# Chunk-selected attention with a top-capacity expert layer: how the gate row reaches all partitions, and how tokens are ranked against it

## What is computed

```python
q, k, v: (4 batches, 8 heads, 768 positions, 64)
ub = sum(max(q * k_min_of_chunk, q * k_max_of_chunk))   # bound per chunk of 32 keys
top_chunks = argsort(where(causal, ub, -1e9))[..., -6:]
mask = sel & (pos[:, None] >= pos[None, :])
attn = softmax(where(mask, 0.125 * q @ k.T, -1e9))
x = (attn @ v) as (3072 tokens, 512)
probs = softmax(x @ w_gate)                  # 8 experts
expert_idx = argmax; gate_w = probs[token, expert_idx]
for e in range(8):
    tok = the 80 tokens of expert e with the largest gate_w
    out[tok] = gate_w[tok] * (relu(x[tok] @ w1[e]) @ w2[e])   # others stay 0
```

## Time and profile before

| | |
|---|---|
| runs | 292.94 us median (291.65 to 294.74) |
| profiled execution | 292.94 us |
| its span | 291.1 us |
| around the span | 1.8 us |
| PE busy | 275.7 us, 95% |
| POOL busy | 226.5 us, 78% |
| DVE busy | 213.7 us, 73% |
| ACT busy | 147.0 us, 51% |
| TensorE clock granted, mean | 0.988 |

### The profile page before, as it was taken

How to read it: one execution, slowest core, us unless ns; L and a number is a source line. 1 busy time by engine, 2 the same in 40 slices (tenths; PEclk the granted TensorE clock), 3 DMA queues, 4 the chain that set the end, 5 groups by cost and what they waited for, 6 DMA issues and landing times.

```text
span 291.1 us, 8693 instructions
## 1 busy us (share of the span) xinstructions
PE 275.7 (95%) x3606; PEld 169.9 (58%) x3609; DVE 213.7 (73%) x575; ACT 147.0 (51%) x202; POOL 226.5 (78%) x295
## 2 busy tenths in 40 slices
PE   7998999999999999999999999999998999885991
PEld 7554656565656565656564657565655675453661
DVE  5897555566978988759889888898899798811341
ACT  2275655555666454645655555656656554321320
POOL 6079899998999999989999999899969950075232
PEclk9999999999999999999999999999999999998997
DMA  9988999999999999999999979999999799416111
GB/s 149 178 141 142 295 173 204 256 173 168 179 159 167 166 184 170 173 153 187 155 168 155 180 136 188 158 187 171 188 315 148 263 148 196 75 55 128 39 59 60
DMA packets 158359, 47.95 MB, mean 165 GB/s; under 512 B 142405, under 2 KB 150721, under 8 KB 158320
## 3 DMA queue, kind: packets, MB, share of 16 engines
q1 hardware_dynamic: 141664, 28.34, 50.2%
q0 software_dynamic: 13520, 18.67, 40.1%
q10 hardware_dynamic: 3136, 0.39, 0.9%
HBM read 53.49 MB, written 11.01 MB: 222 GB/s over the span
## 4 chain that ended last, share of the span: by engine, by line
PE 65%; POOL 19%; DVE 7%; DMA 3%; issue 3%; ACTq 1%; POOLq 0%; ACT 0%; DVEq 0%
PE SC L509 20%; PE OB L568 18%; POOL ES L554 14%; PE SC L524 4%; PE OB L1136 3%; PE M L595 3%; POOL EXB L545 3%; PE OB L641 3%; PE SC L1112 2%; PE M L472 2%; PE M L581 2%; PE MB L497 2%; DMA qn<-in_q_dram 1%; DMA unsT<-in_moe_w_dram 1%; DMA qn<-x_rows,idx 1%
## 5 line engine op out<-in xcount | busy, mean ns | idle before, releaser
L531 ACT ACTIVATE EXB<-SC 128x1024 f32<-128x1024 f32 x96 | 86.3, 917 | 46.4 <-PE SC L524 45.1
L554 POOL TENSOR_TENSOR ES<-ES,EXB 128x256 f32<-128x256 f32 (+1 forms) x105 | 101.7, 980 | 4.8
L509 PE MATMUL SC<-qT,kT 64*128 64x512 f32 (+3 forms) x512 | 96.3, 466 | 0.1
L568 PE MATMUL OB<-EXB,vn 128*64 128x256 f32 (+3 forms) x704 | 73.0, 361 | 2.1 <-POOL EXB L545 2.1
L568 PEld LDWEIGHTS OB<-EXB,vn 128*64 128x64 f32 x704 | 46.8, 137 | 25.6 <-issue 9.8
L509 PEld LDWEIGHTS SC<-qT,kT 64*128 64x128 f32 x512 | 41.4, 186 | 23.0 <-issue 14.3
L554 POOL TENSOR_TENSOR ES<-EXB 128x768 f32<-128x768 f32 (+1 forms) x30 | 46.6, 1554 | 2.5
L524 PE MATMUL SC<-unsT,ind 64*128 64x128 bf16 (+5 forms) x256 | 37.7, 289 | 0.1
L576 ACT ACTIVATE oT<-OB 128x512 f32<-128x512 f32 (+1 forms) x32 | 15.6, 489 | 40.0 <-PE OB L568 40.0
L545 POOL TENSOR_SCALAR_AFFINE_SELECT EXB<-EXB 128x256 f32<-128x256 f32 x79 | 33.8, 437 | 0.5 <-ACT EXB L531 0.5
L524 PEld LDWEIGHTS SC<-unsT,ind 64*128 64x128 bf16 x256 | 12.8, 95 | 17.8 <-issue 8.0
(11 more groups left out here) (222 smaller groups left out, 418.7 us busy)
## 6 DMA issues: line engine op xcount, KB each, us to landing
w1s<-in_moe_w_dram POOLq DMA_DIRECT2D x8, 1024.0 KB, 10.1
w2s<-in_moe_w_dram POOLq DMA_DIRECT2D x7, 1024.0 KB, 10.8
vn<-in_v_dram SPq DMA_DIRECT2D x32, 192.0 KB, 3.3
kn<-in_k_dram SPq DMA_DIRECT2D x62, 96.0 KB, 3.0
qn<-in_q_dram SPq DMA_DIRECT2D x62, 96.0 KB, 4.0
out_dram<-w1s SPq DMA_DIRECT2D x3, 1536.0 KB, 7.9
x_rows<-xp SPq DMA_DIRECT2D x16, 192.0 KB, 3.5
out_dram<-G SPq DMA_DIRECT2D x1, 1536.0 KB, 10.7
```

What stands on the lines that cost most here:

```text
L509: op("pe", lambda: pe.matmul(o, kT[j][pr, ts(kt)], qT[j][pr, q0:q1], start=True, stop=False), r=[f"kT{j}", f"qT{j}"], w=[f"SC{s}"], inc=False)
L531: op("act", lambda: ac.activation(Ex(st, None, 0, W), src, ACTF.Exp, scale=SCALE), r=[f"SC{s}"], w=[f"E{st}"])
L554: op("gp", lambda: gp.tensor_tensor(o, in0, in1, ALU.add), r=[f"E{s2}", f"E{first[0]}"] if first else [f"E{s2}"] + kt, w=kt)
L568: op("pe", lambda: pe.matmul(OB[pr, q0:q1], vn[s][:, kt, h, :], ex, start=(n == 0), stop=last), r=[f"vn{s}{h}", "ES0" if st is None else f ...
```

## The change

Four things change.

1. The gate row of the first three batches. `gt6` gets 32 columns; `row_out` turns it in blocks of 32 on DVE and SP writes the result to DRAM (128 runs of 128 bytes); `row_in` has SP read the 768 gates back, the same 3 KB for each of 128 partitions. `rank_row`, `rank_pred` and `rank_own` are gone.
2. The comparisons. Tiles are no longer rotated; every batch now uses `diag` (six operations), `low` (columns below the tile, "smaller") and `high` (columns above it, "smaller or equal"), and `count` with 24 matmuls of 192 columns.
3. The index tables. There is one integer tile, `tmp_i`, and five of the seven iotas move into `tables`, each waiting until DVE has read the one before.
4. `last_w2` issues its eight loads at once, in step 15 behind the first two selects.

The core of the diff:

```diff
-                vr, vi = iv(144, 128, [E, NT], [1, E]), iv(192, 128, [1, CAP])
-                op("gp", lambda: gp.iota(vr, pattern=[[0, NT], [-1, E]], base=E, channel_multiplier=0), w=["t0"])
...
                 def tables():
-                    op("dve", lambda: ve.tensor_copy(rank_c[:], vr), r=["t0"], w=["rank_c"])
+                    vr = iv(128, [E, NT], [1, E])
+                    op("gp", lambda: gp.iota(vr, pattern=[[0, NT], [-1, E]], base=E, channel_multiplier=0),
+                       r=["ti"], w=["ti"])
+                    op("dve", lambda: ve.tensor_copy(rank_c[:], vr), r=["ti"], w=["rank_c"])
...
+                def row_out():
+                    op("dve", lambda: ve.transpose(gtT[:], gt6[:]), r=["gt6"], w=["gtT"])
+                    o = bass.AP(gd.tensor, gd.offset, [[32, 4], [128, 32], [1, 32]])
+                    op("sp", lambda: sp.dma_start(o, gtT[:]), r=["gtT"], w=["gd"], dsem="d_gd")
+                def row_in():
+                    a = bass.AP(gd.tensor, gd.offset, [[0, 128], [1, S]])
+                    op("sp", lambda: sp.dma_start(G[:, S:2 * S], a), r=["gd"], w=["grow", "growA", "growB"], dsem="d_gr")
...
+                def diag(b, *jts):
                     for jt in jts:
-                        op("dve", lambda: ve.scalar_tensor_tensor(Cl(jt, jt * 128, 128), triQ[:], gt6[:, jt:jt + 1],
+                        op("dve", lambda: ve.scalar_tensor_tensor(Cl(b, jt, jt * 128, 128), triQ[:], gt6[:, jt:jt + 1],
                                                                   G[:, S + jt * 128:S + (jt + 1) * 128], ALU.mult, ALU.is_ge),
-                           r=["triQ", "gt6"] + gk(jt * 128, jt * 128 + 128), w=[f"D{jt}"])
+                           r=["triQ", "gt6"] + gk(jt * 128, jt * 128 + 128), w=[f"D{jt}"] + Cw(b, jt))
...
                     if i == NP - 1:
-                        last_w2(range(4))
+                        last_w2()
                     if live and kk == 1:
-                        rank_pred()
-                        rank_cmp(bb, 5)
+                        low(bb, 5)
                     if live and kk == 2:
-                        rank_count(bb)
+                        count(bb, (5, 0, 4, 1, 3, 2))
                     if live and kk == 0:
                         gate_exp()
                         gate(bb)
+                        row_out()
                     if i + 2 < NP:
                         take_k(i + 2)
+                    if live and kk == 0:
+                        row_in()
                     if i + 4 < NP:
                         load(i + 4, "qk")
                     if live and kk == 1:
-                        rank_diag(bb)
-                        rank_cmp(bb, 4, 3, 2, 1, 0)
+                        diag(bb, *range(NT))
+                        for jt in (0, 4, 1, 3, 2):
+                            if jt:
+                                low(bb, jt)
+                            high(bb, jt)
                     if i + 1 < NP:
                         unselT(i + 1)
-                    if live and kk == 0:
-                        rank_row(bb)
```

More of the change, by code:

```diff
@@ L268, in _body @@
                 lsum = al(pers, "lsum", [128, NT])
-                gt6 = al(pers, "gt6", [128, NT])
+                gt6 = al(pers, "gt6", [128, 32])
+                gtT = al(pers, "gtT", [128, 32])
                 G = al(pers, "G", [128, 2 * S])
@@ L349, in _body, with iv @@
                 M0b = bass.AP(M0, 0, [[512, 128], [1, 512]]).bitcast(BF16)
-                def iv(off, rows, *dims):
-                    return bass.AP(G, off, [[2 * S, rows]] + [list(d) for d in dims]).bitcast(I32)
+                def iv(rows, *dims):
+                    return bass.AP(tmp_i, 0, [[160, rows]] + [list(d) for d in dims])
                 def load(i, what="qkv", eng="sp", gs=range(4)):
@@ L776, in last_count @@
                                                        start=(n == 0), stop=(n == NT - 1)),
[L777 removed]
+                               r=["ohb", f"D{jt}"] + ([f"L{jt}"] if jt else []) + ([f"U{jt}"] if jt < NT - 1 else []) + Cw(b, jt),
                                w=["MB"], inc=(n == NT - 1 and c == 3))
                         keep_warm(warmth[n])
[L781 to L793 removed]
                 def rank_slot(b):
@@ L917, in fill, with last_w2 @@
                     op("sp", lambda: sp.dma_start(zd, zs), r=[zk], w=[f"outz{g}"], dsem=f"d_zero{g}")
-                def last_w2(fbs):
-                    for fb in fbs:
+                def last_w2():
+                    for fb in range(FB):
                         src = bass.AP(moe_w2.tensor, moe_w2.offset + ((E - 1) * Fd + fb * 128) * Dm, [[Dm, 128], [1, Dm]])
@@ L1045, in _body @@
                 values(NP - 1, (1,), (1, 9), False)
-                last_high(0)
-                last_low(5, "act")
+                high(b, 0)
+                low(b, 5, "act")
                 values_out(1)
-                last_low(4, "act")
-                last_low(3, "act")
-                last_diag(0, 1, 2, 3, 4, 5)
-                last_low(1, "dve")
-                last_high(1)
+                low(b, 4, "act")
+                low(b, 3, "act")
+                diag(b, 0, 1, 2, 3, 4, 5)
+                low(b, 1, "dve")
+                high(b, 1)
                 rows(NP - 1)
                 keep_warm(4)
-                last_high(4)
-                last_high(3)
-                last_low(2, "dve")
-                last_high(2)
+                high(b, 4)
+                high(b, 3)
+                low(b, 2, "dve")
+                high(b, 2)
                 scale_rows(NP - 1)
                 gate_gcols(b)
-                last_count((0, 5, 1, 4, 2, 3), (0, 0, 0, 0, 0, 6))
+                count(b, (0, 5, 1, 4, 2, 3), (0, 0, 0, 0, 0, 6))
                 rank_slot(b)
@@ L1158, in _body @@
                 gather(4)
-                last_w2((4, 5))
                 for e in range(1, E):
```

104 lines of the change are left out of this document (33 added, 71 removed).

## The result

The changed kernel takes 311.06 us (median of 4 runs, 309.89 to 311.52) beside 292.29 us (290.05 to 294.74): 1.066 times the time before, 95% interval 1.059 to 1.074. Its profiled execution took 311.52 us with a span of 309.6 us, 18.5 us more than before.

The account below looks back on a forecast made before the run. PE was taken to set the pace, with POOL nearly as busy. Start +3.5, ranks +11.5 and experts -3.8 us sum to +11.2 us: span 302.3, time 304.1, said as 304; the range ran from 293 to 312 us.

Parts of the forecast that it names:

- start: Before step 0's values: five iotas waiting on DVE's table operations delay POOL's first select, and PE; +3.5 us (2.3 to 4.7).
- ranks, first batch: Steps 4 to 6: late row and fifteen comparisons meeting POOL's adds make PE wait 4.8 us at the count; +6.2 us.
- ranks, second: Second batch: SP less behind, row 1.0 us late in place of 2.9, PE's wait at the count 3.9 us; +4.3 us.
- ranks, third: Third batch: POOL waits 2.1 us for a zero fill, during which no add holds DVE; +1.0 us.
- experts: Second weights of expert 7, issued at once: wait and slow matmuls go, select and gather slightly later; -3.8 us (-5 to -2).
- The even odds on the clock: Behind PE's wait at the start, the clock may fall, 1.5 us more for the matmuls; at even odds 0.7 us.
- Comparisons that take 1 to 2 us beside adds: Expected sign on DVE: rank comparisons that meet POOL's adds wait for them and take 1 to 2 us.
- a wait of PE at the count for DVE of 4 to 5 us: Expected sign in step 6, first batch: PE stands 4 to 5 us at the count until DVE's comparisons end.
- less in step 10, little in step 14: Expected sign: PE's wait at the count, 4 to 5 us in step 6, shrinks in the second and third batch.
- DVE hides the fifteen ops: Rival, count in a batch's second step: comparisons end before PE needs them, each batch saves 0.8 us; 290 us, chance 0.14.
- The early loads hold what they should free: Rival, step 15: the eight weight loads hold POOL or the gathers, spending the 3.8 us gain; 308 us, chance 0.20.
- Every row is late: Rival, all three batches: SP stays behind and each batch costs 6.2 us; 311 us, chance 0.16.

Follow-up runs that it names:

- e7: Changed kernel without POOL's adds in steps 6, 10 and 14: 301.35 us beside 292.56 before the change; the profiled run, the fastest of four, took 293.66.
- e3: Changed kernel with the gate row spread by six PE transposes and an ACT copy as before, fifteen comparisons kept: 313.03 us beside 293.45 before the change.
- e6: Changed kernel with sixteen idle 512-column matmuls in front of the count of the first three batches: 302.31 us beside 292.56 before the change.
- e8: Kernel before the change with only the eight last weight blocks issued at once in step 15: 288.71 us beside 292.56, ratio 0.990.
- e2: Changed kernel with the eight last weight blocks issued as before, four, two and two: 316.77 us beside 293.45 before the change.
- e12: Kernel before, with weight blocks at once, row through DRAM, tile 5's comparison and ACT's second row copy moved to the step's end: 292.85 us beside 292.97.
- e1: Changed kernel with the index tables as before, all seven iotas at the program's start: 308.26 us beside 293.45 before the change.
- e4: Kernel before the change with only the gate row transposed on DVE and sent through DRAM by SP: 299.91 us beside 293.45.
- e5: Changed kernel whose first three batches' comparisons no longer wait for each other's writes: 306.31 us beside 292.56 before the change.
- e11: Changed kernel with tables at the start, no write waits between comparisons, first comparison at the step's end, count behind the last scores: 301.83 us beside 292.88 before.
- e9: Changed kernel with the first three batches' count and read-out moved behind the step's last score pieces: 310.13 us beside 292.88 before the change.
- e10: Kernel before, with weight blocks at once, row through DRAM and tile 5's comparison at the step's end: 295.81 us beside 292.88, no interval.

## Why the prediction was right in sign and short in size

304 us was forecast and 311.1 measured: slower, as said, and inside the range. By the prediction's own terms:

| term | predicted | measured, from the table of steps |
|---|---|---|
| start | +3.5 | +3.8 (first sums +4.1, next step -0.2) |
| ranks, first batch | +6.2 | +6.1 (steps 4, 5, 6: -0.65 + 0.8 + 5.9) |
| ranks, second | +4.3 | +6.7 (steps 8, 10: -0.66 + 7.4) |
| ranks, third | +1.0 | +4.75 (steps 12, 14: -0.66 + 5.4) |
| experts | -3.8 | -2.9 (the rest, with the last batch's ranks) |
| sum | +11.2 | +18.5 |

**Start: right in its sum, by two errors that cancel.** PE's wait came out at 2.77 us, 2.0 longer and not 2.8; the 32 matmuls behind it took 1.7 us more, not 0.7. The even odds on the clock were fair: behind waits of 2.76 or 2.77 us these matmuls took 2.82, 2.82, 4.14, 4.30, 4.50 and 5.39 us in six kernels with these tables.

**Ranks: the mechanism was right, the sizes of the second and third batch were not.** "Comparisons that take 1 to 2 us beside adds" and "a wait of PE at the count for DVE of 4 to 5 us" stand in the trace, and e7 and e3's third batch show that the adds do it. The step that failed is "less in step 10, little in step 14". For the second batch the forecast took the lateness of the row as the lever and lowered the wait with it. e3 shows that the row's lateness isn't the lever: with every row in time the ranks of the first two batches end as late against their step. DVE reaches the ranks only when the key reductions are done, and once they pass POOL's first add, three adds hold them however early the row was. For the third batch the forecast relied on POOL's wait for a zero fill. That wait was 1.5 us here, not 2.1, and the first add behind it began while four comparisons were still to come; in e3, where POOL stood longer, step 14 was 3.6 us shorter, so this cover works when it is long enough.

The timelines of DVE split the lateness. Counted from the step's first sums, the ranks end 4.8, 5.3 and 4.6 us later than in the kernel before. Of that the fifteen operations alone are 2.0 us (e7; 1.4 predicted) and a later start 0.4, 0 and 0 us (1.4 predicted in the first batch, 2.9 less the 1.5 on PE). The adds' share is what is left: 2.4, 3.3 and 2.6 us, where 2.5, 2.5 and nothing stood. So the price of the adds was near, and that the first batch came out at +6.1 for +6.2 is in part luck: its row was priced too high, its operations and its clock too low.

The second mis-sized term is the clock. It was priced at 0.7 us, even odds, for each of two batches and at nothing for the third. It fell behind all three counts, and e6 puts it at 1.0, 2.6 and 2.7 us.

The exclusion that the Trainium skill's page "SBUF — State Buffer" gives ("Who interferes with whom"), that the DVE operation and GpSimd's exclude each other for the whole instruction, agrees for the adds: 512 columns took 2.06 us beside one, 0.49 us without. Beside selects it does not show on DVE: the comparisons there took 0.30 to 0.55 us, at most 0.2 us more than their like in e7, and some began in the middle of a select; a select took up to 0.63 us there where it takes 0.41 alone.

**Experts: right, 0.9 us too much.** The blocks alone bring 2 us of the rest in e8 and 3.7 us between e2 and the changed kernel. From the sums of step 15 to the first gather the changed kernel takes 0.8 us longer (0.9 predicted), from there to the end 3.7 us less (4.7 predicted): the wait that goes is the term that was too large. The gather on the chain, 3.80 us, takes part of it back, but not because of the early loads: in e2, without them, it took 3.91.

**The rivals.** "DVE hides the fifteen ops" is refuted by the 13.5 us that PE waits. "The early loads hold what they should free" is refuted by e2 and e8: the gain is not spent. "Every row is late" gave 311 us, the time measured, from a mechanism that did not happen: the rows of the second and third batch were in time. What spoke against it, that PE's waits give SP time, fits: in e7, where PE waits less, DVE waits for all three rows (0.9, 1.2 and 2.8 us). For the first batch it was nearer than the single profile lets one see: the read took 3.9 us in e6 and 9.8 us in e2 from the same place in the program, and the prediction's sentence that the loads behind it "come later ... without being missed" fails in e12.

**When the row lands.** The eleven profiles with the round trip show when its read is slow. In the first batch POOL issues a weight load of 1 MB at about the same time. Where SP issued the read 1.0 to 2.2 us after POOL began on that load, the read took 8.4 to 9.8 us (e1, e2, e4, e5, e11, e12). Where SP issued it earlier than that, up to 0.7 us after, it took 3.9 to 5.1 us (changed, e6, e7, e9, e10). In the second and third batch it went out before the load, or up to 0.3 us after, in all eleven and took 3.3 to 5.0 us. That order holds in all 33 reads; no run moved the read alone or took the load away, so that it is not shown to be the cause.

Not settled: why e7's other runs were longer than its profiled one.

## What to carry to other kernels

Before splitting a vector operation into more pieces, look at what GpSimd does at the time when they will end, not only at their sum: pieces that fit into GpSimd's idle stretch cost their own time (1.5 us here), pieces that run into its adds pay for the adds that they meet (4 to 6 us here, with the clock). A wait of TensorE should be priced with the slow matmuls that may follow: waits of 4.2 to 4.9 us were followed by them in all three batches here, waits of 2.8 us in four of six kernels. Where a transfer can go out right behind a large load, its landing is a range (3.9 to 9.8 us here), and what stands early for it should be able to wait.

## What was not expected of the hardware

Comparisons beside affine selects ran at nearly their own speed, beside adds they did not. And filling PE's wait with idle work (16 matmuls, 3.63 us, no use of their result) made three steps 6.3 us shorter together, though PE had more to do: the granted clock then was 1.00 where it had been 0.50.
